# Six unread filler matmuls of the routing stage give way to 32 unread fp32 matmuls on 32 x 64 tiles of the array

## What is computed

```python
# attention: scores = where(same bucket, q @ k.T / 8, -1e9); softmax; @ v  -> x [1536, 512]
logits = x @ w_gate                       # 8 experts
e_idx = np.argmax(logits, axis=1)
...
for e in range(E):
    mask = e_idx == e
    h = np.maximum(x[mask] @ w1[e], 0.0)
    ye = h @ w2[e]
    out[mask] = gate_w[mask, None] * eom[mask, e, None] * ye
# then: h = out @ w_in; g = elu(h); g @ w_out
```

## Time and profile before

| | us |
|---|---|
| time, median of 2 runs | 767.65 (767.4 to 767.9) |
| span of the profiled execution | 765.7 |
| PE busy | 754.3 (99%) |
| PEld busy | 630.2 (82%) |
| DVE / ACT / POOL busy | 421.5 / 345.6 / 368.7 |
| mean granted clock of TensorE | 0.997 |

### The profile page before, as it was taken

One profiled execution on the slowest core, in us unless ns is written; L12 is line 12 of the kernel. 1 busy time (PEld: TensorE's weight loads), 2 busy tenths in 40 slices (PEclk: granted clock), 3 DMA queues, 4 the chain that ended last, 5 costly groups with the idle time before them and its releaser, 6 DMA issues.

```text
span 765.7 us, 12544 instructions
## 1 busy us (share of the span) xinstructions
PE 754.3 (99%) x4243; PEld 630.2 (82%) x4243; DVE 421.5 (55%) x842; ACT 345.6 (45%) x658; POOL 368.7 (48%) x253
## 2 busy tenths in 40 slices
PE   8999999999999999999999999999999999999996
PEld 7677777777776788888888888998899889989985
DVE  8777777777765645444444545588147126414710
ACT  7766677777764313442244210285047117404610
POOL 5866567878721899777887860244200120010001
PEclk9999999999999999999999999999999999999998
DMA  4534333222111867755675611520200010000000
GB/s 112 128 97 121 92 81 100 57 59 57 28 45 27 324 205 255 219 182 184 213 246 157 233 54 32 194 92 1 61 22 1 29 56 1 0 28 15 1 14 28
DMA packets 42781, 73.70 MB, mean 96 GB/s; under 512 B 20352, under 2 KB 24096, under 8 KB 42720
## 3 DMA queue, kind: packets, MB, share of 16 engines
q1 hardware_dynamic: 29632, 30.05, 13.4%
q10 hardware_dynamic: 9584, 31.53, 12.4%
q0 software_dynamic: 3504, 11.30, 4.6%
HBM read 60.48 MB, written 11.28 MB: 94 GB/s over the span
## 4 chain that ended last, share of the span: by engine, by line
PE 62%; issue 29%; POOL 2%; DVE 2%; ACT 2%; DMA 1%; SPq 0%; POOLq 0%; DVEq 0%
PE pair_s L1478 14%; PE pair_t L1493 14%; PE pair_u L1284 8%; PE bank_b L1299 8%; PE pair_s L1271 5%; PE pair_t L1271 4%; PE pair_u L1453 2%; PE bank_b L1324 1%; POOL out L646 1%; PE pair_s L1531 1%; DVE g_lo L1213 1%; PE bank_a L1240 1%; POOL y_raw L640 1%; POOL w_part L518 1%; PE bank_a L1444 1%
## 5 line engine op out<-in xcount | busy, mean ns | idle before, releaser
L518 POOL TENSOR_TENSOR w_part<-w_raw,w_part 128x1024 fp32r<-128x1024 f32 x80 | 190.2, 2408 | 57.5 <-ACT w_part L756 57.3
L756 ACT ACTIVATE w_part<-w_raw 128x1024 fp32r<-128x1024 f32 x72 | 73.9, 1054 | 126.4 <-PE pair_t L1493 101.4
L1580 PE MATMUL pair_t<-w_part,g_hi 128*128 128x512 f32 x384 | 119.0, 391 | 0.3 <-POOL w_part L518 0.3
L646 POOL DMA_INDIRECT out<-o_sb,token x12 | 11.8, 985 | 208.5 <-DVE o_sb L1183 208.5
L1493 PE MATMUL pair_t<-w_part,hid_t 128*128 x456 | 109.0, 394 | 0.0
L1478 PE MATMUL pair_s<-w_part,xs_t 128*128 x456 | 108.7, 394 | 0.2 <-issue 0.2
L1478 PEld LDWEIGHTS pair_s<-w_part,xs_t 128*128 128x128 f32 x456 | 84.3, 188 | 17.7 <-issue 0.9
L1493 PEld LDWEIGHTS pair_t<-w_part,hid_t 128*128 128x128 f32 x456 | 84.4, 189 | 16.8
L859 ACT ACTIVATE elu<-elu 128x384 f32<-128x384 f32 x64 | 33.6, 525 | 122.9 <-DVE elu L1203 122.8
L698 ACT ACTIVATE exps<-exps,nmax 128x768 f32<-128x768 f32 x96 | 88.5, 925 | 0.6 <-DVE exps L916 0.6
L1580 PEld LDWEIGHTS pair_t<-w_part,g_hi 128*128 128x128 f32 x384 | 71.6, 188 | 15.1 <-issue 0.7
(11 more groups left out here) (219 smaller groups left out, 1088.3 us busy)
## 6 DMA issues: line engine op xcount, KB each, us to landing
w_raw<-in_moe_w ACTq DMA_DIRECT2D x48, 512.0 KB, 6.2
w_raw<-in_moe_w SPq DMA_DIRECT2D x16, 512.0 KB, 5.6
ys_sorted<-ys SPq DMA_DIRECT2D x19, 256.5 KB, 3.6
w_raw<-in_moe_w_in ACTq DMA_DIRECT2D x8, 512.0 KB, 5.7
raw<-in_q SPq DMA_DIRECT2D x16, 192.0 KB, 3.1
raw<-in_k SPq DMA_DIRECT2D x16, 192.0 KB, 3.3
v_nat<-in_v SPq DMA_DIRECT2D x16, 192.0 KB, 2.6
x_rows<-rows_sb SPq DMA_DIRECT2D x32, 96.0 KB, 2.3
```

Of the source, the lines that this page charges most:

```text
L518: pool.tensor_tensor(chunk_of(w_part, n, 1, c), w_raw[n % 2][c][:, :], chunk_of(w_part, n, 0, c).bitcast(F32), ALU.subtract).then_inc(s_wl ...
L756: act.activation(chunk_of(w_part, n, 0, c), w_raw[n % 2][c][:, :], ACT.Copy).then_inc(s_whi, 1)
L1580: mm = pe.matmul(pair_t[:, t % 2, :], gp[:, f, j * P:(j + 1) * P], w_out_p[:, wp, f, :], start=f == 0 and m == 0, stop=f == FT - 1 and m == 2)
```

## The change

The third number of `WARM` goes from 16 to 10. Behind `warm(2)` two calls of a new function issue 16 matmuls each, two rounds over eight tiles. A tile is 32 rows (r) by 64 columns (o) of the array. The first call takes both column halves of a row group before it goes to the next row group; the second takes the four row groups of one half and then those of the other. The operands are the same weights in `w_part`, read as plain fp32, 192 columns moved; the outputs go to 192 columns in each of four banks, one bank for a row group, and nobody reads them. All of it stands ahead of the waits for `s_tab`, `s_cnt` and `s_src`. Nothing else is changed.

```diff
-WARM = (10, 14, 16, 3)
+WARM = (10, 14, 10, 3)
...
+            def warm_tiles(rounds, rows_first):
+                for _ in range(rounds):
+                    for i in range(8):
+                        o, r = (i % 2, i // 2) if rows_first else (i // 4, i % 4)
+                        rows = slice(r * 32, (r + 1) * 32)
+                        bank = (pair_s, pair_t)[r // 2][o * D:(o + 1) * D, r % 2, 0:192]
+                        pe.matmul(bank, w_part[rows, 0, 1, 0:D].bitcast(F32), w_part[rows, 0, 0, 0:192].bitcast(F32),
+                                  start=True, stop=True, tile_position=(r * 32, o * D))
+
             warm(2)
+            warm_tiles(2, True)
+            warm_tiles(2, False)
             pe.wait_ge(s_tab, 1)
             pe.wait_ge(s_cnt, 1)
             pe.wait_ge(s_src, 1)
```

## The result

The changed kernel took 776.37 us (two executions, 776.07 and 776.66) against 767.65 us: a ratio of 1.0113, interval 1.0094 to 1.0132. The forecast was 768.4 us with a range of 767.1 to 771.4. Its profiled execution spans 774.3 us, 8.6 more than before, and stands 1.8 us under its own time.

A forecast was written before the change was run, and what follows sets the result against it. TensorE, busy 99% of a 765.7 us span, was taken as the bound. Removed fillers 0, later transposes +0.7, gave a 766.4 us span; with 1.95 us to the median, 768.4 us, range 767.1 to 771.4.

The forecast's parts named there:

- Removed fillers: Six fillers under the gather of x, 1.37 us of TensorE work, go at no gain; the tenth starts at 249.35.
- The tiles: Before the transposes of x, eight tiles work side by side: 64 passes in eight rounds, 1.33 us, hidden under the gather.
- The rival of row tiles that wait for each other: Tile passes run four, two or one at once: +1.5, +3.5 or +8.6 us; chances 0.08, 0.12 and 0.04.
- one-at-once case: Tile passes run one after another, transposes of x at 260.1, +8.6 us, 776.3 us; chance 0.04.
- The sequencer: Slot-table reads wait until all but 17 passes have left the queue; transposes at 252.1, +0.7 us (+0.45 to +1.2).
- nothing moves: Sequencer hands over faster or holds more than 17 passes, so reads end before 251.4: 767.7 us; chance 0.16.
- the hand-over in part 4: Before the slot-table reads, handing over 47 passes takes about 0.025 us each (0.033 at most); sequencer free at 250.7.
- None is late, so nothing is given back: Behind the transposes, POOL's gathers, SP's weight loads and DVE's gate arithmetic don't wait for TensorE and stay in place.
- what delays TensorE at 251 us delays the end one for one: From the routing stage on, TensorE's chain is unbroken and later waits move with it, so the +0.7 us reaches the end.
- The clock: TensorE idles before the transposes and its clock halves for up to about 3 us: 1.5 us lost, 769.9 us; chance 0.08.
- The theory of supply: Theory at the start of the experiments: 64 closely packed passes outrun the sequencer's side, so the last 17 come late.

The follow-up runs named there:

- e1_no_tiles: The changed kernel without its 32 tile matmuls, so only the six fillers are gone: 767.75 us, ratio 1.0.
- e13_changed_again: The changed kernel run again with no edit, on another chip: 768.37 us over 9 executions, ratio 1.0012.
- e8_dve_first: The changed kernel with DVE's small operations for the output rows moved ahead of its copies of x: 771.79 us, ratio 1.0061.
- e5_cols_once: The changed kernel without its first tile call, leaving 16 matmuls (32 passes) of the second call: 769.02 us, ratio 1.0017.
- e11_bf16_cols: The changed kernel with 64 one-pass bf16 tile matmuls, all in the second call's order, in place of its fp32 ones: 768.12 us, ratio 1.0007.
- e3_small_bf16: The changed kernel with 64 whole-array bf16 matmuls of 16 moved columns in place of the tiles: 769.4 us, ratio 1.0034.
- the swapped kernel: The changed kernel with its two tile calls in the other sequence: 776.56 us, ratio 1.0119, two executions of 781.83 and 771.29.
- e14_rows_again: The changed kernel with all 64 passes in the first call's order, repeated on chip D: 767.31 us, ratio 1.0003.
- e10_early: The changed kernel with all 64 passes in the second call's order, placed ahead of the ten fillers: 767.55 us, ratio 1.0003.
- e2_half: The changed kernel with only the first tile call, 16 matmuls or 32 passes: 767.76 us, ratio 1.0008.

## Why the prediction was wrong, step by step

**Removed fillers: right.** The tenth starts at 249.34 against the forecast 249.35, and without them nothing is lost (`e1_no_tiles`).

**The tiles: right.** Row tiles work side by side. Eight tiles start within 0.05 us, rounds 0.16 us apart; in `e13_changed_again` the last starts 1.23 us after the first (249.73 to 250.96), so with its 0.16 us of streaming the run ends after 1.39 against the 1.33 of the sum. The rival of row tiles that wait for each other falls, as do its times; that its one-at-once case said 776.3 us is chance, since there the transposes would have come at 260.1 and not at 255.3.

**The sequencer: right where nothing was held up, wrong in the first measurement.** On chips A, C, D and E it is free with 15 or 16 of the 64 fp32 passes left, then reads, and the transposes follow; the prediction's 250.7 to 250.8 for the wait and the read is what `e13_changed_again` shows. The transposes came 0.97 us later than in the kernel before against a forecast of 0.7, within its bounds (+0.45 to +1.2): the two reads took 1.5 us from 250.8 to 252.3, where the sum took the 1.3 of the next slot and not the 1.4 of this one. The rival "nothing moves" falls with it: in every kernel with 64 passes just ahead of the reads the transposes came later, and the ratio of the changed kernel is above 1 in both repetitions (1.0002 at least). Such a delay reaches the end almost whole, as the forecast had it. Compared among executions that have the two late waits and a full clock, the spans with 64 fp32 passes ahead of the reads are 766.6 to 767.0 against 765.7. The kernel of the first order alone shows how the groups blur this: it has 1.0004, 1.0003 and 1.0013 on three chips, with five, six and none of its executions in the faster group, while within each group it is 0.8 to 1 us above the kernel before.

**The step that failed** is the hand-over in part 4. The sum took 0.02 to 0.033 us for a pass handed over, set the sequencer free at 250.7 and bounded the delay of the transposes at +1.2. In the first measurement the first 47 passes had started by 250.83, near that pace. The last 17 started from 251.35 to 253.8, and the sequencer was free at 253.6, not with 17 passes left but with 4 or 5: 2.9 us that the sum didn't have. It was the same in the three profiles of chip B that were held up (4 or 5 left at 253.4 to 253.9). Nothing in the trace of before shows such a pause; the widest tiled stretch there has 12 passes. Why the hand-over slowed down stays open (below).

**"None is late, so nothing is given back": the forecast looked at the wrong work.** I asked whether POOL's and SP's work stays in place, and it does, within some tenths: POOL's first operation on the weights starts at 257.49 before and at 257.98 after. I did not ask what DVE's work, which does move, would then lie beside. DVE's block had 0.85 us of room before POOL's operation at 257.49 (it ended at 256.64). A shift of 0.97 fits because POOL's operation also came later there (258.48); a shift of 3.9 puts the block under three of POOL's operations, and that costs 3.29 us more. `e8_dve_first` shows it by moving the block. So "what delays TensorE at 251 us delays the end one for one" was wrong for a delay of this size.

The Trainium skill, "SBUF — State Buffer", section "Who interferes with whom", says that a DVE operation with two SBUF inputs contends with a GpSimd operation that reads SBUF, that copies, casts and scalar operations contend with GpSimd when they run in a two-port mode, that the loser blocks fully, and that a reduce never does. The trace agrees in the main: the add L1153 and the cast L1159 ended with POOL's operations, while the reduce L1152 ran in 0.25 us at 258.19, under the same operation of POOL that then held L1153. Whether the cast ran in a two-port mode, no run shows.

**The clock: right rival, wrong weight.** It was priced at +1.5 us with a chance of 0.08 and as a case by itself. In the first measurement it came on top of the others: +1.25 and +1.46 us, each over 3.4 us at 0.50 granted, close to the forecast's "up to about 3 us long, 1.5 us lost". The cases were put side by side as if only one could happen, while a late start brought the hold on DVE with it (`e8_dve_first`), and half clock came more often with a hold-up: in three of its four profiles, and in two of the 15 others (`e5_cols_once`, `e11_bf16_cols`). With them chained, the range should have reached past 771.4.

**What stays open.** Why the last 17 passes are handed over 2.9 us late on chip B and in the first measurement. Excluded as the sole cause: the order of tiles (chips B and D), and the number of passes (`e3_small_bf16` and `e11_bf16_cols` on A and C, the tile kernels on D and E). That it belongs to the chip fits, since every kernel with 64 such passes was held up on chip B and none on the four others, but it was not shown. Chip B has two or four executions of each such kernel and one profile, the two of the swapped kernel were 10.5 us apart, the changed kernel itself was never run there, and no single kernel was profiled both ways on one chip. The theory of supply is not excluded for that chip; that the sequencer was late itself speaks for something on its side. In `e5_cols_once`, also on chip B, no pass was held, but the work that waits for TensorE began 1.3 us late. A delay in TensorE's reports of completion would fit both, if the sequencer waits for such reports before it hands over more; no run tells it from late delivery of instructions.

The Trainium skill, "Runtime: NRT & Kernel Launch", section "Instruction fetch mechanics", says that instructions come in blocks of 16 KB, and that fetching them is hidden because dispatch is slower. By the trace one such packet was moved at 250.98 us in the held execution and took 1.22 us. In `e13_changed_again` one was moved at 250.67 and took 1.37, and in `e14_rows_again` one at 251.06 took 1.71, with no hold-up, so no run here ties the two together.

## What to carry to other kernels

When one engine's block is moved later, list what it will then run beside: DVE's small operations cost 0.2 us alone and 3 us beside POOL's, and a shift of 0.97 us cost no more than itself where one of 3.9 us cost twice its size. Where the sequencer has to read a value, put few and long matmuls in front of it (`e10_early`: the same 64 passes ahead of ten fillers cost nothing), since with 64 short ones it is free only when some 17 are left. And measure a change near 1% more than once and in more than one place: here one file took 776.4 us and 768.4 us, while the kernel before agreed within 0.2 us everywhere. Look at single times beside the median: a kernel whose executions fall in two groups shows differences of up to a microsecond that are only a matter of how many fall in each.

## What the runs showed of the hardware that I had not expected

- Tiles of 32 rows by 64 columns start 6 to 8 ns apart in fp32, eight to a round of 0.16 us, and mostly 3 or 4 ns apart in bf16 (`e11_bf16_cols`). On the whole array 64 small bf16 matmuls started 25 ns apart (`e3_small_bf16`).
- At its wait the sequencer was 17 ahead with one-pass bf16 matmuls on the whole array and 15 or 16 with 64 fp32 tile passes, but 24 with 32 of them (`e2_half`, `e5_cols_once`) and 8 with bf16 tile passes (`e11_bf16_cols`). No single number describes it.
- The end of a densely packed run of tile passes came 2.9 us late, in bursts 0.7 us apart, in four kernels, with the sequencer 4 or 5 passes ahead at its wait, and not at all in the same or nearly the same kernels on four other chips.
- A DVE operation on 12 or 19 columns took 1.95 to 3.06 us while POOL ran an elementwise operation on 1024 columns, against 0.17 or 0.18 us in the kernel before.
- With DVE's block moved (`e8_dve_first`) the granted clock of the profiled execution stayed at 1.00 although TensorE's own thin stretch was the same.
